# Probabilities normalised on GpSimd before their transposes, with a pipeline that is two slots longer

## The reference

```python
# 1: attention that keeps the 32 largest scores of a row
scores = q @ k.T / 8                      # (576, 576) for each batch and head
kth    = 32nd largest of each row
scores = where(scores >= kth, scores, -1e9)
attn   = exp(scores - max(row));  attn /= sum(row) + 1e-9
x      = concat over heads of attn @ v
# 2: gated convolution
gate   = sigmoid(causal 5-tap depthwise conv of x)
x      = (gate * (x @ w_val)) @ w_out
# 3: real part of the 2-D Fourier transform, added to x; layer norm;
#    then relu(un @ w_ch1) @ w_ch2, added
```

## Time and profile before

| quantity | value |
|---|---|
| median of 3 runs | 1215.79 us (1215.04 to 1216.76) |
| the profiled execution's own time | 1214.56 us |
| its span in the profile | 1212.8 us |
| PE busy | 1049.4 us (87%) |
| DVE busy | 884.3 us (73%) |
| ACT busy | 621.3 us (51%) |
| POOL busy | 406.9 us (34%) |
| mean granted TensorE clock | 0.926 |

### The profile page before, as it was taken

One profiled execution on the slowest core, in us unless ns is written; L12 is line 12 of the kernel. 1 busy time (PEld: TensorE's weight loads), 2 busy tenths in 40 slices (PEclk: granted clock), 3 DMA queues, 4 the chain that ended last, 5 costly groups with the idle time before them and its releaser, 6 DMA issues.

```text
span 1212.8 us, 19844 instructions
## 1 busy us (share of the span) xinstructions
PE 1049.4 (87%) x6608; PEld 841.9 (69%) x6608; DVE 884.3 (73%) x1898; ACT 621.3 (51%) x1253; POOL 406.9 (34%) x704
## 2 busy tenths in 40 slices
PE   3776565789798989989798989999798999998998
PEld 2554454666587878866587878775587888648887
DVE  6999999996996978696996978696996970330000
ACT  3786766644565655554565655454565653012221
POOL 2444533142443332233433332322443322133221
PEclk9886756889898999999898999999898999998999
DMA  8566455021355856321355846321365655206974
GB/s 256 163 202 203 140 187 188 11 74 35 102 209 193 282 192 198 134 75 46 111 217 192 270 178 213 123 70 45 126 226 202 226 179 204 108 1 237 351 277 162
DMA packets 81188, 200.37 MB, mean 165 GB/s; under 512 B 8384, under 2 KB 26560, under 8 KB 81088
## 3 DMA queue, kind: packets, MB, share of 16 engines
q1 hardware_dynamic: 81088, 199.11, 48.2%
HBM read 177.58 MB, written 21.50 MB: 164 GB/s over the span
## 4 chain that ended last, share of the span: by engine, by line
PE 56%; issue 14%; DVE 12%; POOL 10%; ACT 5%; DMA 1%; SPq 1%; DVEq 0%; ACTq 0%; POOLq 0%
PE p_m L567 15%; PE p_m L553 15%; PE p_m L461 14%; DVE rest L742 5%; PE p_t L434 4%; PE p_t L450 4%; PE p_s L421 4%; DVE top L748 3%; ACT prob L630 2%; POOL k_lo L876 2%; POOL bias L884 1%; POOL hid_lo L949 1%; POOL w_st L901 1%; POOL bias L885 1%; DMA u<-w_ch 1%
## 5 line engine op out<-in xcount | busy, mean ns | idle before, releaser
L748 DVE MAX8 top<-rest 128x8 f32<-128x576 f32 x432 | 304.7, 747 | 0.0
L949 POOL TENSOR_TENSOR hid_lo<-hid,hid_hi 128x256 fp32r<-128x256 f32 (+1 forms) x128 | 107.0, 836 | 325.8 <-ACT hid_hi L692 325.8
L742 DVE MATCH_REPLACE8 rest<-top,rest 128x576 f32<-128x576 f32 x288 | 211.7, 743 | 0.0
L553 PE MATMUL p_m<-un_hi,w_st 128*128 128x320 f32 (+1 forms) x1024 | 172.9, 313 | 44.6 <-POOL un_lo L940 25.3
L567 PE MATMUL p_m<-w_st,hid_hi 128*128 128x512 f32 x640 | 206.3, 404 | 0.2 <-POOL hid_lo L949 0.2
L553 PEld LDWEIGHTS p_m<-un_hi,w_st 128*128 128x128 f32 x1024 | 149.6, 198 | 55.5 <-POOL un_lo L940 26.2
L630 ACT ACTIVATE prob<-s_sb,bias 128x576 f32<-128x576 f32 x144 | 111.1, 772 | 105.0 <-POOL bias L885 104.6
L623 ACT ACTIVATE s_sb<-p_s 128x576 f32<-128x576 f32 x144 | 93.1, 646 | 136.3 <-PE p_s L421 136.2
L434 PE MATMUL p_t<-id_sb,prob 128*128 128x128 f32 x720 | 122.1, 306 | 34.4 <-ACT or_sb L652 34.0
L421 PE MATMUL p_s<-k_hi,q_st 128*128 128x512 f32 (+1 forms) x320 | 118.2, 372 | 33.2 <-POOL k_lo L876 19.5
L450 PE MATMUL p_t<-pT,v_sb 128*64 128x128 f32 (+1 forms) x1600 | 106.9, 285 | 43.5 <-ACT pT L643 23.4
(11 more groups left out here) (78 smaller groups left out, 1602.9 us busy)
## 6 DMA issues: line engine op xcount, KB each, us to landing
w_st<-w_split SPq DMA_DIRECT2D x256, 512.0 KB, 4.4
w_split<-w_st SPq DMA_DIRECT2D x32, 512.0 KB, 3.0
q_raw<-qT SPq DMA_DIRECT2D x64, 144.0 KB, 3.4
k_raw<-kT SPq DMA_DIRECT2D x64, 144.0 KB, 3.4
u<-w_ch SPq DMA_DIRECT2D x32, 256.0 KB, 3.6
v_sb<-v SPq DMA_DIRECT2D x16, 256.0 KB, 3.5
wslot<-w_val SPq DMA_DIRECT2D x4, 1024.0 KB, 5.3
wslot<-w_out SPq DMA_DIRECT2D x4, 1024.0 KB, 5.3
```

Of the source, the lines that this page charges most:

```text
L553: mm = pe.matmul(mbank(HIDDEN_BANK[g], n), w1_st[i % NB1][:, w, k, :], x[:, k, at:at + n], start=part + k == 0, stop=part + k == KC + 1)
L742: dve.match_replace(rest[tt % 2][:, :], top[tt % 4][:, 8 * n - 8:8 * n], src[:, :], LOWEST).then_inc(s_chain, 1)
L748: found = dve.max(top[tt % 4][:, 8 * n:8 * n + 8], rest[tt % 2][:, :])
L949: pool.tensor_tensor(hid_lo[i % 2][:, 0:WIDTH[g]], hid[:, 0:WIDTH[g]], hid_hi[i % 2][:, 0:WIDTH[g]].bitcast(F32), ALU.subtract).then_inc(m ...
```

## The change

The division by the row sum moves from behind the attention product to ahead of the transposes. POOL multiplies each tile of probabilities (128x576, in place) by its reciprocal in a new `normalise(t)`, and PE's transposes wait for that. The four reciprocal matmuls, the `or_sb` buffer and `scale_out` go; `store_out` writes the output straight to `x_new`. `EXPONENT` becomes 5, `TRANSPOSE` 8 and `ATTEND` 9, `RECIP` stays 6; `prob` gets four buffers, and the small lists (`top`, `bias`, `psum_row`, `rinv`) eight. Batch steps start two slots later. In the step list "trn 0" and "trn 1" come earlier ("trn 0" ahead of "seq 2", "trn 1" ahead of "proj 4"), and the first two layer norms are issued on DVE after "proj 1" and "proj 2". Some convolution and tanh slots move by one or two.

```diff
-STEPS += [..., ("proj", 3), ("seq", 2), ("trn", 0), ("proj", 4), ("trn", 1)]
+STEPS += [..., ("proj", 3), ("trn", 0), ("seq", 2), ("trn", 1), ("proj", 4)]
-NORM_AT = {("proj", 2): 0, ("seq", 2): 1, ("ch0", 1): 2, ("ch0", 4): 3, ("ch0", 7): 4}
+NORM_AT = {("proj", 1): 0, ("proj", 2): 1, ("ch0", 1): 2, ("ch0", 4): 3, ("ch0", 7): 4}
-SELECT, EXPONENT, RECIP, TRANSPOSE, ATTEND = 1, 4, 6, 6, 7
+SELECT, EXPONENT, RECIP, TRANSPOSE, ATTEND = 1, 5, 6, 8, 9
+NP = 4
...
                 def transpose_p(t):
-                    pe.wait_ge(s_exp, t + 1)
+                    pe.wait_ge(s_norm, t + 1)
...
                     if t and unit_due(t + TRANSPOSE - 1):
-                        pe.wait_ge(s_or, unit_of(t + TRANSPOSE - 1 - ATTEND) + 1)
+                        pe.wait_ge(s_x, unit_of(t + TRANSPOSE - 1 - ATTEND) + 1)
...
                 def attend(t):
-                    pe.wait_ge(s_rinv, t // 2 + 1)
...
-                    for h, (tt, c0) in enumerate(src):
-                        mm = pe.matmul(p_o[D * h:D * h + D, 1, 0:n],
-                                       rinv[:, tt % 4:tt % 4 + 1].broadcast_to((P, D)),
-                                       id_sb[:, c0:c0 + n], start=True, stop=True, skip_group_check=True)
...
                 def store_out(t):
-                    act.activation(or_sb[n_u % 2][:, :, 0:n], p_o[:, :, 0:n], ACT.Copy).then_inc(s_or, 1)
+                    act.activation(x_new[p % NX][:, at:at + n], p_o[:, 0:n], ACT.Copy).then_inc(s_x, 1)
...
-                def scale_out(t):
...
-                    pool.tensor_tensor(x[:, at:at + n], src[:, 0, 0:n], src[:, 1, 0:n], ALU.mult).then_inc(s_x, 1)
+                def normalise(t):
+                    pool.wait_ge(s_rinv, t // 2 + 1)
+                    p = prob[t % NP][:, 0:S]
+                    pool.tensor_scalar(p, p, rinv[:, t % NK:t % NK + 1], None, ALU.mult).then_inc(s_norm, 1)
...
                     for x in plan[s][0:1]:
                         step(*x)
-                    if unit_due(s):
-                        scale_out(s - ATTEND)
                     for x in plan[s][1:]:
                         step(*x)
+                    if due(s, RECIP) and (s - RECIP) % 2:
+                        normalise(s - RECIP - 1)
+                        normalise(s - RECIP)
```

More of the change, by code:

```diff
@@ L21 @@
 NS = 6
-FILLS = 17
+FILLS = 18
 TOPK = 32
+NK = 8
 SCALE = 1.0 / float(np.sqrt(D))
@@ L68 @@
 STEPS = [("val", j) for j in range(2 * KC)] + [("zed", m) for m in (2, 0, 1)]
-STEPS += [("seq", 0), ("proj", 0), ("proj", 1), ("seq", 1), ("proj", 2), ("proj", 3), ("seq", 2), ("trn", 0), ("proj", 4),
-          ("trn", 1)]
+STEPS += [("seq", 0), ("proj", 0), ("proj", 1), ("seq", 1), ("proj", 2), ("proj", 3), ("trn", 0), ("seq", 2), ("trn", 1),
+          ("proj", 4)]
 for f in range(FC + 1):
@@ L142, in build @@
         rest = [sb(f"rest{i}", [P, S]) for i in range(2)]
[L143 to L147, removed]
+        top = [sb(f"top{i}", [P, TOPK]) for i in range(NK)]
+        bias = [sb(f"bias{i}", [P, 2]) for i in range(NK)]
+        prob = [sb(f"prob{i}", [P, SP]) for i in range(NP)]
+        psum_row = sb("psum_row", [P, NK])
+        rinv = sb("rinv", [P, NK])
         pT = [sb(f"pT{i}", [P, NCH, P]) for i in range(3)]
-        or_sb = [sb(f"or_sb{i}", [P, 2, P]) for i in range(2)]
         x_new = [sb(f"x_new{i}", [P, XW]) for i in range(NX)]
@@ L627, in exponent @@
                     act.wait_ge(s_bias, 2 * (t + 1))
[L628 to L633, removed]
+                    if t >= NP:
+                        act.wait_ge(s_tr, t - NP + 1)
+                    act.activation(prob[t % NP][:, 0:S], s_sb[t % NS][:, :], ACT.Prelu,
+                                   bias=bias[t % NK][:, 1:2], scale=-BIG, alpha=1.0 / BIG).then_inc(s_drop, 1)
+                    if t >= NK:
+                        act.wait_ge(s_radd, (t - NK) // 2 + 1)
                     act.wait_ge(s_drop, t + 1)
-                    act.activation(prob[t % 3][:, 0:S], prob[t % 3][:, 0:S], ACT.Exp,
-                                   bias=bias[t % 4][:, 0:1], scale=-SCALE,
-                                   accum_out=psum_row[:, t % 4:t % 4 + 1]).then_inc(s_exp, 1)
+                    act.activation(prob[t % NP][:, 0:S], prob[t % NP][:, 0:S], ACT.Exp,
+                                   bias=bias[t % NK][:, 0:1], scale=-SCALE,
+                                   accum_out=psum_row[:, t % NK:t % NK + 1]).then_inc(s_exp, 1)
                 def store_pT(t):
@@ L741, in select @@
                             src = s_sb[tt % NS] if n == 1 else rest[tt % 2]
-                            dve.match_replace(rest[tt % 2][:, :], top[tt % 4][:, 8 * n - 8:8 * n], src[:, :],
+                            dve.match_replace(rest[tt % 2][:, :], top[tt % NK][:, 8 * n - 8:8 * n], src[:, :],
                                               LOWEST).then_inc(s_chain, 1)
@@ L747, in select @@
                             dve.wait_ge(s_chain, done[tt])
-                            found = dve.max(top[tt % 4][:, 8 * n:8 * n + 8], rest[tt % 2][:, :])
+                            found = dve.max(top[tt % NK][:, 8 * n:8 * n + 8], rest[tt % 2][:, :])
                             if n == TOPK // 8 - 1:
@@ L842, in step @@
                         normalise(b, NORM_AT[what, n])
-                for i in range(3):
+                for i in range(NP):
                     dve.memset(prob[i][:, S:SP], 0.0).then_inc(s_zero, 1)
```

50 lines of the change are left out of this document (22 added, 28 removed).

## The result

The changed kernel takes 1387.4 us (median of 4 runs, 1386.1 to 1388.6) against 1215.7 us for the kernel before: a ratio of 1.141, with a 95% interval of 1.139 to 1.143. The direction and the wait that I named are right. The size is not: +172 us where I had forecast +48.5, and 85 us above the upper end of the range.

A forecast was written before the change was run, and what follows sets the result against it. The prediction took DVE to bound the start and PE the batches; 15.5 (start) + 14 + 14 + 8 (batches) - 3 (last stage) = +48.5 us on 1214.6 gave 1263 us, 1264 on the median's scale, range 1224 to 1302 us.

The forecast's parts named there:

- the list: PE's waits in a batch, slot by slot, mostly for normalise at POOL's slot end: 45.2 us against 20.3 before.
- The rival that the lag hides normalise: In the batches the eight-slot lag keeps POOL ahead, PE never waits at an even slot: 1183 us, chance 0.10.
- part of the waits: Rival: waits behind "proj", "seq" and "val" stand, those of hidden steps are hidden by PE's sums: some 1240 us, chance 0.22.
- Two slots more at the start: Steps start two slots later, so two more slots run at DVE's pace, one a split slot: +11.5 us.
- The wait of 7.2 us: PE's wait for the layer norm's low part at a batch's first hidden step, to become about 1.0 us.
- Reciprocal matmuls: Taking them out saves PE 5.9 us a batch where PE sets the pace, nothing at the start.
- the 6 credited: Third batch: nine slots instead of seven run without scores at its end, credited with a gain of 6 us.
- step 1: Price of one normalise on POOL: slope of two-input products halved, 0.8 us, bounds 0.2 and 1.39 us.
- the rival: Normalise at the two-input price, 1.39 us: +25 us in the batches, +12 at the start, 1300 us, chance 0.13.
- step 2: New ring through ACT, POOL and PE in slots 8 to 33: 10.6 us for two slots against DVE's 9.9; +4 us.
- step 3: Batches: waits less matmuls give +19 us, a full-speed walk +11, half-clock stretches partly covered; +14 taken, +8 for the third.
- step 4: How normalise holds up PE in the batches: PE's transposes wait for POOL's normalise at the end of odd slots.

The follow-up runs named there:

- e2_norm_first: The changed kernel with POOL's two normalise moved right behind the biases of the odd slot, ahead of weight split and steps: 1219.2 us, ratio 1.004.
- e3_schedule_only: The kernel before with the changed kernel's lags, buffers, small lists and order of steps, but the old arithmetic (no normalise on POOL): 1220.0 us, ratio 1.006.
- e8_order_only: The kernel before with only the new order of steps and norms, lags and arithmetic as before: 1197.6 us, ratio 0.987.
- e1_norm64: The changed kernel with normalise on only 64 of 576 columns of each tile, its place kept: 1295.8 us, ratio 1.067.
- e6_lag9: The changed kernel with TRANSPOSE 9, ATTEND 10, five prob buffers and the last two pairs' convolution and tanh slots one later: 1319.4 us, ratio 1.087.
- e9_lag9_bias_first: e6_lag9 with POOL issuing the next slot's biases ahead of the two normalise in odd slots, except before a split slot: 1240.8 us, ratio 1.022.
- e12_first_norm64: e2_norm_first with normalise on only 64 of 576 columns of each tile: 1208.9 us, ratio 0.996.
- e4_norm_dve: The changed kernel with normalise on DVE, right behind its two reciprocals, instead of on POOL: 1251.6 us, ratio 1.031.

## Why the prediction was right and wrong

**Right: the mechanism.** PE's largest wait is at the transposes, released by normalise, for the reason given: normalise behind that slot's steps. e2_norm_first shows it, by taking only the place away. Place by place the waits are near the list, if one allows each of them 1 us more because normalise is that much longer: 4.0 us behind "proj 0" (2.9 predicted), 6.6 behind "proj 2" (5.8), 4.5 behind "seq 2" and "trn 1" (3.7). Behind the first two "val" halves it was 3.8 us, less than the 5.2 predicted and only the fifth longest. The rival that the lag hides normalise (1183 us) is refuted, and so is "part of the waits": at hidden steps, too, PE waits.

**Near the forecast: the small terms.** Two slots more at the start: +12.0 us in e3_schedule_only, 11.5 predicted (8.2 against e8_order_only, whose start is that of the kernel before but for the spread). Last stage: -5.0, -3 predicted. The wait of 7.2 us became 1.0 us, as predicted. Reciprocal matmuls: PE's busy time in the second batch falls from 248.9 us (e3_schedule_only) to 243.2 (e2_norm_first), 5.7 us for 5.9, though the mean granted clock rose from 0.96 to 0.97 between them, so not all of it need be the matmuls. Third batch without normalise: -6.1 us. That equals the 6 credited by luck, since the forecast also counted the 6.2 us of the first hidden step there. Against e8_order_only, with the same order of steps, the longer pipeline gains 2.1 us in this batch.

**Wrong, step 1: "I halve the slope: 0.8 us", with 1.39 us as upper bound.** It took 1.78 us. The premise that one input must be cheaper than two doesn't hold on this engine: from 128x64 to 128x576 it grows by 1.25 us over 512 columns, 2.4 ns a column, against 2.1 for the products with two inputs. The upper bound was a belief about the operation and not a row. What a tenth of a microsecond is worth was near the mark: (310.6 - 290.2) / 12.5 = 1.6 us a batch (1.4 predicted), and at the start 25.9 / 12.5 = 2.1 us (2.0 predicted, from the 12 us for 0.6 in the rival). Put on the straight line through e1_norm64 and the changed kernel, 0.8 us gives an estimate of 1295.8 + 0.27 x 73.3 = 1316 us. So of the 123 us that I was off, the price is some 71, and 52 are the steps that follow.

**Wrong, step 2: "A slack of one slot absorbs part of some 9 us; I take +4 us".** Of the start's +63.8 us the two slots are 12, so the ring costs 52; at a price of 0.8 us still 32. POOL, first stage of the changed kernel, one pair of slots:

```profile
189.87 3.47 POOL L888 TENSOR_SCALAR prob<-prob,rinv 128x576 f32<-128x576 f32 x2
193.43 0.22 POOL L882 TENSOR_SCALAR bias<-top 128x1 f32<-128x1 f32 x1
193.74 0.48 POOL L883 TENSOR_SCALAR bias<-top 128x1 f32<-128x1 f32 x1
...
196.60 1.28 POOL L893 TENSOR_TENSOR w_st<-u,w_st 128x512 fp32r<-128x512 f32 x1 [2.37 <-ACT w_st L659]
197.97 0.22 POOL L882 TENSOR_SCALAR bias<-top 128x1 f32<-128x1 f32 x1
198.27 0.31 POOL L883 TENSOR_SCALAR bias<-top 128x1 f32<-128x1 f32 x1
...
201.31 1.27 POOL L893 TENSOR_TENSOR w_st<-u,w_st 128x512 fp32r<-128x512 f32 x1 [2.73 <-ACT w_st L659]
202.55 3.98 POOL L888 TENSOR_SCALAR prob<-prob,rinv 128x576 f32<-128x576 f32 x2
```

From one pair of normalise to the next it takes 12.7 us, where DVE's two slots take 9.9. POOL waits for ACT's weight copy; that stands behind the exponential; that waits for the biases; and these stand on POOL behind *both* normalise. I had put one normalise and PE's transposes into my ring and reached 10.6 us. In this stretch PE's way is just not the last: ACT's store of the transposed tile, which stands ahead of the exponential, ends at 193.7 us and the biases at 194.2. Elsewhere it has a share. From the first pair of normalise to the fifteenth it takes 201.0 us in the changed kernel, 184.7 in e6_lag9 (direct way open), 155.3 in e9_lag9_bias_first (the biases ahead of normalise too, the weight split still in front of it) and 162.7 in e2_norm_first. So the ring through the biases is shown as the larger part. With normalise at the front 9.7 us of the start's loss stay beyond e3_schedule_only, 5.4 of which go when it is 0.53 us long (e12_first_norm64).

**Wrong, step 3: "which a new wait may partly cover ... I take +14".** My list of waits was sound: 45.2 us a batch predicted, 55.2 us of idle PE measured, with 1 us more of price at fourteen places. But I then took 5 us off the +19 that the list gave, for half-clock stretches that waits might cover. The waits did the reverse: the granted clock went from 0.96 to 0.92, and PE's busy time rose by 6.3 us where the removed matmuls were to take 5.9 away. e2_norm_first has the same matmuls without most of the waits, and is busy 243.2 us at 0.97 instead of 255.5 at 0.92. On the straight line between e1_norm64 and the changed kernel the second batch at a price of 0.8 us would be 290.2 + 0.27 x 16.3 = 294.6 us, +25 (an estimate): as much as the +24.9 of waits, with the 5.9 us of matmuls lost to the clock.

**Wrong, step 4, which only e6_lag9 shows in the batches: normalise's ways to PE.** I looked at the one that goes through `s_norm`. The one through the next slot's biases, ACT's exponential and `store_out` was not in the walk. With the direct way open it alone keeps the first two batches at 292 to 296 us; with both open they take 274 to 275.

**Taken too high: the gain at the first hidden step.** My sum takes "1.0 instead of 7.2" as a gain of the whole batch. In e3_schedule_only nothing of it is left: other waits of PE took its place, as the rows above show. In e8_order_only the second batch is 6.6 us shorter, so it is the lags, not the order, that take it back; why is open, as said above.

## What to carry to other kernels

Before an operation is given to an idle engine, list what stands in front of it *and behind it* in that engine's order, and follow both to the leading engine: here the same operation, 1.78 us long in both, left the kernel 0.4% slower in one place and 14% in another. A pipeline's lag in slots is full slack only for what stands at the front of a slot: here one slot more of lag and the next biases ahead of normalise gave back 147 of the 172 us with normalise left at the end. And an upper bound needs a row of that operation on that engine; where there is none, carry the range past the nearest row.

## What the runs showed of the hardware

- GpSimd's product of a tile with a value per partition (float32, in place) took 0.47 us at 64 columns, 0.63 at 128 (from the identity into another tile) and 1.75 at 576 (medians; means 0.53, 0.64 and 1.78). VectorE took 0.52 us for the last (mean 0.69, longest 1.65). The Trainium skill ("GPSIMD Engine Reference", Engine selection) calls a one-input operation there roughly line-rate; this case's traces don't agree, at 2.4 ns a column and 3.4 times VectorE's time by the medians. Its advice against elementwise work on GpSimd isn't what decided: e4_norm_dve, with the product on VectorE, is 32 us slower than e2_norm_first, with it on GpSimd.
- A float32 128x128 transpose is one matmul record of TensorE, a float32 product of the same size two of the same length (720 records, 307 ns mean; 1440, 302).
- A change that makes TensorE wait also makes its work longer: with 5% fewer records in the second batch its busy time rose 2.5%, as the mean granted clock fell from 0.96 to 0.92.
